# Attention and two MLP layers on one core: one row-maximum chunk in each step of a head

## What is computed

```python
q_bits = (q @ proj > 0); k_bits = (k @ proj > 0)        # 6 bits each
mask = bucket(q_bits)[:, None] == bucket(k_bits)[None, :]
scores = where(mask, q @ k.T / sqrt(64), -1e9)          # 16 heads, 768 x 768
attn = exp(scores - max(scores)); attn /= sum(attn) + 1e-9
x = (attn @ v)  ->  1536 tokens x 512
h = x @ w_in;  x = (max(h, 0) + alpha * min(h, 0)) @ w_out
h = x @ w_in2; out = (P(h) / (Q(h) + 1e-6)) @ w_out2    # P cubic, Q quadratic
```

## Time and profile before

| what | value |
|---|---|
| median of 3 runs | 846.24 us (844.61 to 846.59) |
| profiled execution, its time | 847.52 us |
| its span | 845.4 us |
| granted TensorE clock over the span | 0.992 of full speed |
| busy share: TensorE, VectorE, ScalarE, GpSimd | 96%, 68%, 50%, 33% |
| attention | up to about 292 us of the span |
| MLP | from 294.5 us on |

### The profile page before, as it was taken

How to read it: one execution, slowest core, us unless ns; L and a number is a source line. 1 busy time by engine, 2 the same in 40 slices (tenths; PEclk the granted TensorE clock), 3 DMA queues, 4 the chain that set the end, 5 groups by cost and what they waited for, 6 DMA issues and landing times.

```text
span 845.4 us, 11501 instructions
## 1 busy us (share of the span) xinstructions
PE 810.8 (96%) x3665; PEld 647.1 (77%) x3665; DVE 575.8 (68%) x886; ACT 418.8 (50%) x639; POOL 282.2 (33%) x365
## 2 busy tenths in 40 slices
PE   8899999999999799999999999998999999999996
PEld 5667777877778678888888888886788788887884
DVE  5578778788877445335433444459998888879885
ACT  1566768777777601112011211136676666667663
POOL 5366556636645599500000044554600000000000
PEclk9999999999999989999999999999999999999999
DMA  6465665565654253200000012212100100010001
GB/s 171 111 164 151 174 155 139 153 167 132 176 125 119 70 158 111 74 1 0 1 1 1 0 51 75 64 61 75 50 1 1 50 0 0 0 50 1 1 1 50
DMA packets 34408, 60.96 MB, mean 72 GB/s; under 512 B 10076, under 2 KB 12612, under 8 KB 34372
## 3 DMA queue, kind: packets, MB, share of 16 engines
q1 hardware_dynamic: 34372, 60.49, 26.0%
HBM read 29.51 MB, written 3.19 MB: 39 GB/s over the span
## 4 chain that ended last, share of the span: by engine, by line
PE 55%; DVE 5%; ACT 2%; issue 2%; DMA 1%; ACTq 0%; DVEq 0%
PE ps_h L1022 28%; PE acc L1040 27%; DVE work L1179 1%; DVE num L1183 1%; DVE num L1167 1%; DMA out<-stage 1%; DVE work L1173 1%; ACT work L1097 1%; DVE den_q L1160 1%; ACT work L1094 1%; DVE g_lo L1144 0%; DVE num L1163 0%; DVE x_lo L1192 0%; ACT g_hi L1074 0%; ACT work L1083 0%
## 5 line engine op out<-in xcount | busy, mean ns | idle before, releaser
L1074 ACT ACTIVATE g_hi<-num 128x512 fp32r<-128x512 f32 x96 | 60.9, 634 | 219.4 <-PE acc L1040 200.1
L1150 DVE TENSOR_SCALAR num<-ps_h,alpha_sb 128x512 f32<-128x512 f32 x48 | 36.0, 751 | 137.0 <-PE ps_h L1022 137.0
L796 DVE TENSOR_REDUCE row_max<-ps_a 128x1 f32<-128x384 f32 x192 | 97.7, 550 | 24.4 <-PE ps_a L430 23.5
L576 ACT ACTIVATE ps_s<-ps_s 128x768 f32<-128x768 f32 x96 | 76.5, 796 | 65.8 <-PE ps_s L473 65.4
L824 DVE TENSOR_TENSOR p_lo<-ps_s,p_hi 128x768 fp32r<-128x768 f32 x96 | 90.9, 948 | 10.6 <-ACT p_hi L583 10.6
L583 ACT ACTIVATE p_hi<-ps_s 128x768 fp32r<-128x768 f32 x96 | 77.8, 811 | 3.4
L1144 DVE TENSOR_TENSOR g_lo<-num,g_hi 128x512 fp32r<-128x512 f32 x96 | 73.5, 766 | 8.2 <-ACT g_hi L1074 1.4
L1022 PE MATMUL ps_h<-x_hi,w_late_in_hi 128*128 128x512 f32 (+1 forms) x288 | 78.9, 396 | 0.0
L1022 PE MATMUL ps_h<-x_hi,w_late_in_lo 128*128 128x512 f32 (+1 forms) x288 | 78.8, 396 | 0.0
L1022 PE MATMUL ps_h<-x_lo,w_late_in_hi 128*128 128x512 f32 (+1 forms) x288 | 78.8, 395 | 0.0
L1082 ACT ACTIVATE den_q<-ps_h,abs_b 128x512 f32<-128x512 f32 x48 | 33.1, 689 | 84.9 <-PE ps_h L1022 70.1
(11 more groups left out here) (133 smaller groups left out, 1759.7 us busy)
## 6 DMA issues: line engine op xcount, KB each, us to landing
stage<-in_w_in SPq DMA_DIRECT2D x26, 256.0 KB, 2.8
stage<-in_w_out SPq DMA_DIRECT2D x26, 256.0 KB, 3.0
raw<-in_qk SPq DMA_DIRECT2D x16, 384.0 KB, 3.1
q<-hi SPq DMA_DIRECT2D x32, 192.0 KB
k<-hi SPq DMA_DIRECT2D x32, 192.0 KB
v_raw<-in_v SPq DMA_DIRECT2D x16, 192.0 KB, 3.0
qa<-hi SPq DMA_DIRECT2D x16, 192.0 KB
ka<-hi SPq DMA_DIRECT2D x16, 192.0 KB
```

The lines of the kernel that those rows point to most:

```text
L576: nc.scalar.activation(p32, p32, ACT.Exp, scale=float(D) ** -0.5).then_inc(s_exp, 1)
L796: dve.tensor_reduce(row_max[slot][:, i, c:c + 1], ps_a[:, i, 0:HALF], AX.X, ALU.max).then_inc(s_a_free, 1)
L1074: nc.scalar.activation(g_hi[f % 2][:], num[f % 4][:], ACT.Copy).then_inc(s_ghi, 1)
L1150: dve.tensor_scalar(num[f % 4][:], h, 0.0, alpha_sb[:, f:f + 1], ALU.min, ALU.mult).then_inc(s_step, 1)
```

## The change

The table of extra work is laid out anew: each step of a head from 1 on has exactly one row-maximum chunk, and they all belong to head h+2, so that a head finds its own chunks done when it starts. The bits move to step 0, the turn to step 1. Head 0, which must catch up, gets three chunks in each of its last two steps. VectorE does `low` first in every step, then all uses. The counts on the semaphores, until now formulas, are taken from one list that walks the table. ScalarE's `split_v` moves from step 1 to 2, `x_high` from step 4 to 3 (odd heads), `stat_rows` from 2 to 1 with the turn. GpSimd does `normalise` ahead of `split_v`, and `x_low` ahead of `split_qk`.

```diff
-                more, bits = left > 0, left > 1 or (left == 1 and u == 0)
-                return [([("a", 1, 4)], [("a", 1, 5)]),
-                        ([], [("bits", 3, 0)] if bits else []),
-                        ([("m", 1, 0)], []),
-                        ([], [("a", 2, 0)] if more else []),
-                        ([("a", 2, 1)] if more else [], [("a", 2, 2)] if more else []),
-                        ([], [("a", 2, 3)] if more else [])]
+                return [([("bits", 3, 0)] if bits else [], [("a", 2, 0)] if more else []),
+                        ([("m", 1, 0)], [("a", 2, 1)] if more else []),
+                        ([], [("a", 2, 2)] if more else []),
+                        ([], [("a", 2, 3)] if more else []),
+                        ([], [("a", 2, 4)] if more else []),
+                        ([], [("a", 2, 5)] if more else [])]
...
# head 0, its last two steps
-                            ([("a", 2, 0)], [("a", 2, 1)]),
-                            ([("a", 2, 2)], [("a", 2, 3)])]
+                            ([("a", 2, 0)], [("a", 2, 1), ("a", 2, 2)]),
+                            ([("a", 2, 3)], [("a", 2, 4), ("a", 2, 5)])]
...
             def turn_step(j, u):
-                return 3 if isinstance(j, int) and j + u == 0 else 2
+                return 3 if isinstance(j, int) and j + u == 0 else 1
...
# counts: a list of what is done when, in place of formulas
+            def use_counts():
+                done, pair_start, n = {}, [], 0
+                for kind, g, c in FIRST:
+                    n += 2
+                    done[kind, g, c] = n
+                for h in range(HEADS):
+                    if h % 2 == 0:
+                        pair_start.append(n)
+                    left = min(2, PAIRS - 1 - h // 2)
+                    for before, after in uses_of(left, h % 2, h == 0):
+                        for kind, g, c in before + after:
+                            n += 2
+                            done[kind, h + g, c] = n
+                return done, pair_start
...
# ScalarE
-                            if c == 1 and not (final and u == 1):
+                            if c == 2 and not (final and u == 1):
                                 split_v(1 - u, j + u)
-                            if c == 4 and u == 1 and not first:
+                            if c == 3 and u == 1 and not first:
                                 x_high(act, j - 1)
...
# GpSimd
                             row_stats(1 - u, h + 1)
+                        if u == 1 and not (isinstance(j, int) and j == 0):
+                            normalise(j - 1)
+                        if not (final and u == 1):
                             split_v(1 - u, h + 1)
                         if isinstance(h, int) and h == 0:
                             bit_rows(0, 1)
                             split_qk(0, 1)
-                        if u == 1 and not (isinstance(j, int) and j == 0):
-                            normalise(j - 1)
                         if left > 1 or (left == 1 and u == 0):
                             bit_rows(1 - u, j + 1 + u)
-                            split_qk(1 - u, j + 1 + u)
                         if u == 1 and not (isinstance(j, int) and j == 0):
                             x_low(j - 1)
+                        if left > 1 or (left == 1 and u == 0):
+                            split_qk(1 - u, j + 1 + u)
...
# VectorE
-                            for kind, g, cc in steps[c][0]:
-                                if kind != "m":
-                                    use(kind, (u + g) % 2, j + (u + g) // 2, cc, n)
-                                    n = n + 2
-                            if c == 3 and not (final and u == 1):
-                                sum_parts(1 - u, j + u)
-                                n = n + 2
                             if c + 1 < KC or not (final and u == 1):
                                 low((c + 1) % KC, t + 1)
+                            for kind, g, cc in steps[c][0] + steps[c][1]:
+                                at = (u + g) % 2, j + (u + g) // 2
+                                if kind == "m":
+                                    sum_parts(*at)
+                                else:
+                                    use(kind, *at, cc, n)
+                                n = n + 2
+                                if kind == "a" and cc == KC - 1:
+                                    maxima(*at, n)
```

More of the change, by code:

```diff
@@ L219, in halves @@
                 return t.rearrange("p (n c) -> p n c", n=2)
-            FIRST_USES = 2 + KC + 1 + 4 + 1
             USES = KC + 2
@@ L256, in a_chunks_done, with uses_done @@
+            DONE, PAIR_START = use_counts()
+            MIDDLE = HEADS // 2
+            def uses_done(kind, g, c):
+                if isinstance(g, int):
+                    return DONE[kind, g, c]
+                return 2 * USES * g + (DONE[kind, MIDDLE, c] - 2 * USES * MIDDLE)
             def a_chunks_done(g):
-                return 2 * (KC + 2) if isinstance(g, int) and g == 0 else 2 * USES * g + 2 * (FIRST_USES - USES + 2)
+                return uses_done("a", g, KC - 1)
             def bits_done(g):
-                if isinstance(g, int) and g < 4:
-                    return 2 * (1, 2, FIRST_USES + 2, FIRST_USES + 4)[g]
@@ L264, in bits_done @@
-                return 2 * USES * g + 2 * (FIRST_USES - 3 * USES + 3)
+                return uses_done("bits", g, 0)
             def turned(g):
[L269 to L278, removed]
+                return uses_done("m", g, 0)
@@ L280, in over_pairs, with halves_before @@
+            def halves_before(j):
+                if isinstance(j, int):
+                    return PAIR_START[j]
+                return 4 * USES * j + (PAIR_START[2] - 8 * USES)
             def over_pairs(eng, body):
@@ L340, in load_raw @@
                     else:
-                        sp.wait_ge(s_a_out, 2 * USES * g - (12 * USES - bits_done(4)))
+                        sp.wait_ge(s_a_out, 2 * USES * g - (2 * USES * (MIDDLE + 2) - bits_done(MIDDLE)))
                     sp.dma_start(raw[u][:], qk[bass.ds(g, 1)].rearrange("a p s -> (a p) s")).then_inc(s_raw[u], 16)
@@ L524, in pair @@
                     final = not left
-                    n = halves_before(j, left)
+                    n = halves_before(j)
                     for u in range(2):
```

## The result

The changed kernel took 839.8 us (median of 5 runs, 839.08 to 841.86) against 846.24 us (median of 5, 844.61 to 849.24). The ratio is 0.9927 with a 95% interval of 0.9911 to 0.9943, so it is faster by 6.2 us by the ratio and by 6.4 by the medians, where 8.9 was forecast. The profiled execution took 839.08 us.

What follows compares the result with a forecast made beforehand. TensorE was taken as the bound, its score weight loads waiting 17.9 us for VectorE's p_lo. Heads 2 to 12 -10.9, head 13 +0.7, head 0 +1.8, head 1 -0.5: -8.9 from 846.24 gives 837.3 us, range 832.5 to 843.5.

Steps and rivals of the forecast that it cites:

- head 0: First attention head: two more chunks to take, 3 a step on VectorE at 0.93 us each, +1.8 us.
- head 1: Second attention head: turn waits for GpSimd's mcols behind the weight split, 15.44 + 0.4 against 16.34 us, -0.5 us.
- head 14: Last attention head: loses two chunks but waits for the landing of den as before, 1.92 us idle, change 0.
- TensorE's steps: Each head: step 0 3.69 us, step 1 3.00, steps 2 to 4 2.10 each, step 5 2.45, sum 15.44.
- The reciprocals: After step 2 of even heads: both operations take 0.4 us, delaying low for step 4; 0.3 us a head.
- rival B: Even heads: reciprocals collide with pen or stall low in full, 1.1 us instead of 0.3, total 842.1 us; chance 0.17.
- Step 1: Turn's step: chunk waits until ScalarE's copy and sum_parts free ps_a; 3.00 us, bounds 2.5 and 3.1.
- The fill: SyncE's copies for chunk 0, wanted in step 0, land late behind store and spread: 0.2 us in odd heads, 1.8 in head 13.
- double step: Two-chunk step before the change: VectorE needs 2.72 us against TensorE's 2.45; 0.6 us of each step is a wait.
- A: Rival: the new waits vanish (turn's step at 2.5 us, no reciprocal stall, no fill wait), 828 us; chance 0.13.
- D: Rival: slower, because the fill becomes the bound and odd heads wait for chunk 0, 850.5 us; chance 0.05.
- the moved side work: Reordered ScalarE and GpSimd work: hidden, cost 0; without cover ScalarE's two copies cost up to 1.6 us per odd head.

Runs made afterwards that it cites:

- change: The changed kernel measured again without an edit, beside the kernel before: 842.58 us, ratio 0.9949.
- recip_early: Changed kernel, but VectorE does the reciprocals of an even head ahead of step 2's reductions instead of behind them: 844.07 us, 0.9971 of the kernel before.
- stat_first: Changed kernel, but ScalarE copies the turn's result ahead of the step's exponential instead of behind it: 841.75 us, 0.9947 of the kernel before.
- spread_late: Changed kernel, but SyncE issues the fill of the next chunks between the store of the reciprocals and their spread: 838.62 us, 0.9906 of the kernel before.
- double_back: Changed kernel, but step 2 of a head gets two row-maximum chunks again and the next step none: 847.96 us, 1.0013 of the kernel before.
- old_side: Changed kernel's table and VectorE order, with ScalarE's and GpSimd's work ordered as in the kernel before: 840.12 us, 0.9919 of the kernel before.
- last_recip: Changed kernel, but in head 14 VectorE does the reciprocals after step 3, not step 2: 839.94 us, 0.9928 of the kernel before.
- turn_after: Changed kernel, but the turn moves behind step 1's values, its chunk ahead of them, and ScalarE copies the turn first in step 2: 843.95 us, 0.9969.
- best: Changed kernel with the fill issued between store and spread, and head 14's reciprocals after step 3: 837.31 us, 0.9901 of the kernel before.

## Why the prediction was right, and where not

By the stretches of the two profiles the forecast holds up as follows: heads 2 to 12 -8.7 us (forecast -10.9), head 0 +2.1 (+1.8), head 1 -0.8 (-0.5), head 13 -0.3 (+0.7), head 14 -0.3 (0), together -7.9 against -8.9. The medians moved by 6.4 only, because the profile of before lay 1.3 us above its median and that of the changed kernel 0.7 below. Part of the agreement is luck: heads 2 to 12 fell short by 2.2 us, and head 13 gave 1.0 of it back.

- **TensorE's steps.** Forecast 3.69, 3.00, 2.10, 2.45 and 15.74 us for an even head; measured 3.67, 3.01, 2.10, 2.44 in head 6, and 15.70 to 15.77 in heads 4, 6, 8 and 10. Consecutive single-chunk steps, which no row of before showed, run at TensorE's pace as worked out.
- **The reciprocals.** Forecast 0.3 us a head; steps 3 and 4 of head 6 are 2.29 and 2.21 where 2.10 is bare: 0.3. That L118 escapes `pen` came out with nothing to spare: in heads 4 to 10 it starts 0.02 to 0.08 us before `pen` ends and takes 0.16 to 0.17. In head 12 `pen` started later, at +8.9 us instead of +8.3, and L118 took 0.60 us; step 3 took 2.78 and the head 16.19. In the profile of `change` it was 1.16 us there. `recip_early` shows the lock and rival B's price of 0.8 us. The Trainium skill, SBUF — State Buffer, section "Who interferes with whom", says that a VectorE operation in a mode that uses both SBUF ports (`tensor_scalar` can) and a GpSimd operation contend, and that the one issued first blocks the other for its whole length. The traces agree: wherever L118 started 0.5 us or more before the end of `pen`, 20 times in five profiles, it ended 0.03 us after `pen`.
- **Step 1.** The size was right, the reason half right: head 0's row gave the +2.54, but `stat_first` shows that the copy's place behind the exponential is not what sets it. The turn itself is late: its second part waits 0.3 us a head for the reductions (3.2 us in 12 places), and only 0.2 us of the forecast 0.4 is left as L444's wait for `v_sum` (2.5 us in 13).
- **The fill.** Forecast 0.2 us in odd heads: mis-sized. They took 15.52, 16.18, 15.87, 16.15 and 15.78 us, 15.90 in the mean where 15.64 was forecast, 1.3 us in all. Head 13 waited 0.8 us in the first profile and 1.6 in `change`, forecast 1.8. A slack of 0 worked out from one head is a coin toss; `spread_late` removed it.
- **Heads 2 and 12** took 0.5 us more each. In head 2 the turn waited 0.7 us for `mcols`: the weight split of head 1 reaches that far, which I had counted for head 1 alone. Head 12 is the late `pen` above.
- **Head 0** lost 2.1 us, forecast 1.8. Its first four steps are 1.3 us faster with the new order (step 4 starts at 42.94, not 44.22), and that is lost again in a wait of 1.73 us for the stats' copy, 0.38 before. The two rows, before and after:

```profile
45.22 0.61 PE L473 MATMUL ps_s<-q,k 128*128 128x384 f32 x2 [0.38 <-DMA q<-stats]
```

```profile
45.29 0.62 PE L487 MATMUL ps_s<-q,k 128*128 128x384 f32 x2 [1.73 <-DMA q<-stats]
```

- **Head 14** is the term whose mechanism was wrong. It was put at 0 because the wait for `den` stays. It was 0.25 us shorter with the clock up and 1.4 longer with it down. The landing of `den` keeps its place, 8.6 us into the head, and TensorE reaches the wait 0.9 us sooner than before, so its gap grew. Before, and after in the first profile:

```profile
276.14 0.59 PE L468 MATMUL ps_s<-q,k 128*128 128x384 f32 x2 [1.12 <-DVE p_lo L824]
```

```profile
268.29 0.58 PE L482 MATMUL ps_s<-q,k 128*128 128x384 f32 x2 [1.75 <-DVE p_lo L840]
```

Nine profiles are of kernels with the new table in which the reciprocals keep this place in head 14. In six of them the gap is 1.75 to 1.85 us, and in four of these six the clock fell behind it (heads of 15.5 us). In the other three the gap is 1.24 to 1.46 us, and it fell in none (heads of 13.8 to 13.9 us, as in the two where it stayed up). With head 0, where the same happened, this is 3.0 of the 3.5 us between the profiles of 839.1 and 842.6 us. I had looked at that wait and asked only whether it stayed, not how long TensorE would stand.

- **What the argument missed.** It put the 0.6 us of a double step down to VectorE's 2.72 us against 2.45. `double_back` and the new steps bear out that such a step costs 0.5 us and more, though by another wait once `low` comes first: the second chunk's for the first one's reductions. But it never asked what the new order would do to the old table, and that gives half of the gain in heads 2 to 12 and, without head 0's extra chunks, the same median. With the order alone an odd head takes 16.0 us, in the changed kernel 15.5 where no fill waits. The double steps (2.83 and 3.18 us where 2.45 is bare) cost 1.1 us more than need be; the new table saves that and pays 0.5 of it for the chunk in the turn's step (3.01 where 2.49 is bare). So the even spread is worth about 4 us in heads 2 to 12 and pays 2.4 of it back in head 0, or 3.7 where the clock falls there. The new table with VectorE's old order was not run, so the table's worth by itself stays open.
- Of the rivals, A was refuted (step 1 stays at 3.0), and D did not come about. B's time is close to the 842.6 us of `change`, but its mechanism is not: L118 took 0.16 to 0.17 us in heads 2 to 10 of both profiles. By the time alone `old_side` confirms that the moved side work counts for nothing.

## What to carry to other kernels

When an engine's order and a table of work change together, price each alone: here `low` first would have given the same for one reordered loop. When the critical engine gets faster, look at each wait that is tied to something else (a DMA's landing, another engine's long operation): it now stands longer, and in these profiles gaps of 1.6 to 1.9 us cost the clock on top in some executions. Between a store and the read that must wait for it, let the queue issue something that nobody is early for.

## What was not expected of the hardware

TensorE's clock after a gap in attention. The wait for the stats' copy in head 0 took 1.51 to 2.00 us in the eleven profiles of kernels with the new table. The clock fell from 2.4 to 1.2 GHz behind it in three, after 1.61, 1.77 and 1.90 us (`last_recip`, `turn_after`, `change`), and stayed up in eight, one of them after 2.00 us (`stat_first`). It was low for some 3 us in `change` and for nearly 7 in the other two. In head 14 it fell in four of the six profiles with 1.75 to 1.85 us. After the 1.12 us in head 14 of before it stayed up. Even the 3.1 us ahead of the MLP did not always lower it: granted 0.50 for some 7 us in the profile of before, for some 3 in the first of the changed kernel, and never in those of `stat_first` and `best`.

A VectorE addition on 12 numbers a partition took 0.17 us alone and 0.93 to 1.24 us when it started inside a GpSimd operation, always ending 0.03 us after it.
